# Zeros for 128 rows per expert once all tokens are counted, places read straight from TensorE's counts, and all gates computed at the end

## Time and profile before

| | us |
|---|---|
| runs | 1171.95, 1174.45, 1176.95 (median 1174.45) |
| the profiled execution, device time | 1172.36 |
| its span, first to last instruction | 1170.7 |
| TensorE busy | 1045.8 (89%) |
| VectorE busy | 577.0 (49%) |
| ScalarE busy | 484.0 (41%) |
| GpSimd busy | 306.9 (26%) |

### The profile page before, as it was taken

The page is one execution under the profiler, slowest core; times in us unless marked ns, Lnnn a source line. Parts: engine busy times, 40 slices in busy tenths (PEclk is TensorE's granted clock), DMA queues, the critical chain, the costliest instruction groups (busy, mean ns, idle before and its releaser), DMA issues.

```text
span 1170.7 us, 15177 instructions
## 1 busy us (share of the span) xinstructions
PE 1045.8 (89%) x4960; PEld 738.7 (63%) x4961; DVE 577.0 (49%) x1140; ACT 484.0 (41%) x1094; POOL 306.9 (26%) x309
## 2 busy tenths in 40 slices
PE   4999798897209999999999999499999999999998
PEld 3667575574204444444444444389999999999997
DVE  3775867757401111111111111697777777777764
ACT  5776666663100111111111111575555555555554
POOL 5665655743020000000000000432323232232222
PEclk9999999998658999999999999699999999999999
DMA  8554554505691444103491110200101000010000
GB/s 204 133 141 137 157 140 139 146 23 157 247 369 47 180 180 165 50 34 130 170 373 37 36 36 18 63 2 1 54 1 54 1 24 32 1 55 1 28 1 27
DMA packets 52758, 110.95 MB, mean 95 GB/s; under 512 B 7256, under 2 KB 16472, under 8 KB 52184
## 3 DMA queue, kind: packets, MB, share of 16 engines
q1 hardware_dynamic: 44104, 87.35, 23.5%
q0 software_dynamic: 4992, 16.26, 4.3%
q10 hardware_dynamic: 3600, 6.56, 1.4%
HBM read 82.36 MB, written 27.79 MB: 94 GB/s over the span
## 4 chain that ended last, share of the span: by engine, by line
PE 66%; DVE 2%; issue 1%; DMA 1%; POOL 1%; ACT 0%; POOLq 0%; DVEq 0%
PE scores L1294 15%; PE average L1302 15%; PE scores L1345 5%; PE scores L1347 5%; PE scores L1346 5%; PE average L1360 2%; PE mix L1361 2%; PE turned L1360 2%; PE scores L1309 2%; PE average L1361 2%; PE turned L1361 2%; PE mix L1360 2%; PE average L1359 2%; PE turned L1359 2%; PE mix L1359 2%
## 5 line engine op out<-in xcount | busy, mean ns | idle before, releaser
L1294 PE MATMUL scores<-w_sb,xt 128*128 x400 | 178.6, 600 | 2.3 <-issue 1.4
L1302 PE MATMUL average<-w_sb,hidt 128*128 x400 | 175.9, 593 | 1.0 <-DVE hidt L1009 1.0
L526 POOL TENSOR_TENSOR g_lo<-g,g_hi 128x384 fp32r<-128x384 f32 x96 | 98.2, 1023 | 290.4 <-ACT g_hi L728 290.4
L1345 PE MATMUL scores<-yt_hi,w_in_hi 128*128 128x384 f32 x384 | 132.4, 345 | 1.2 <-DVE yt_lo L1030 1.2
L1294 PEld LDWEIGHTS scores<-w_sb,xt 128*128 128x128 f32 x400 | 75.1, 193 | 88.2 <-issue 88.2
L1347 PE MATMUL scores<-yt_hi,w_in_lo 128*128 128x384 f32 x384 | 130.2, 339 | 0.0
L1346 PE MATMUL scores<-yt_lo,w_in_hi 128*128 128x384 f32 x384 | 130.0, 339 | 0.0
L1302 PEld LDWEIGHTS average<-w_sb,hidt 128*128 128x128 f32 x400 | 74.1, 190 | 84.9 <-issue 84.9
L1051 DVE COPY_PREDICATED ser<-big,th 128x384 f32<-128x384 int32 x96 | 118.8, 1238 | 3.3
L683 ACT ACTIVATE hid<-scores 128x512 f32<-128x512 f32 x50 | 29.9, 597 | 218.1 <-PE scores L1294 218.1
L1004 DVE COPY xt<-turned 128x512 f32<-128x512 f32 x26 | 18.0, 692 | 206.0 <-PE turned L1284 206.0
(11 more groups left out here) (231 smaller groups left out, 2077.6 us busy)
## 6 DMA issues: line engine op xcount, KB each, us to landing
w_sb<-in_w SPq DMA_DIRECT2D x14, 2048.0 KB, 13.8
q_sb<-in_qt SPq DMA_DIRECT2D x48, 288.0 KB, 4.1
x_sorted<-zeros SPq DMA_DIRECT2D x8, 1408.0 KB
k_sb<-in_kt SPq DMA_DIRECT2D x32, 288.0 KB, 4.3
xin<-x_sorted POOLq DMA_DIRECT2D x26, 256.0 KB, 2.9
y_sorted<-y_sb ACTq DMA_DIRECT2D x25, 256.0 KB, 2.0
v_sb<-in_v SPq DMA_DIRECT2D x16, 256.0 KB, 2.6
w_sb<-in_w SPq DMA_DIRECT2D x8, 512.0 KB, 3.8
```

The lines of the kernel that those rows point to most:

```text
L526: pool.tensor_tensor(g_lo[:, t % GRING, :], g32[:, t % 2, :], g_hi[:, t % GRING, :].bitcast(F32), ALU.subtract).then_inc(g_lo_ok, 1)
L1294: last = mm(s_ps[0][j][:, :], xt[:, c, :], w1_sb[:, r, c, j * 512:(j + 1) * 512], start=c == 0, stop=c == CD - 1)
L1302: last = mm(o_ps[0][:, :], hidt[:, c, :], w2_sb[:, r, c, :], start=c == 0, stop=c == CF - 1)
L1345: mm(ff_h(t), w_h, yt_hi[:, j % 2, c, :], start=c == 0, stop=False)
```

## The change

- `fill` writes 128 rows for each expert instead of 704, in one DMA with one row for each partition. It runs once all four batches are counted (`r_fill`, set after the last batch's rows), not after three.
- GpSimd scatters the last batch without waiting for the fills; the wait for `filled` stands behind these scatters, ahead of the tile loads.
- SyncE loads w1 of expert 1 once x is complete, then come the fills, then w2 of expert 1 and both of expert 2.
- All `turn_x` of a batch stand at the end of a step: tiles 0 and 1 at i = 4 of half 0, tile 2 at i = 3 and tiles 3 and 4 at i = 4 of half 1. ScalarE copies all five. The scores of i = 2 and 3 in half 1 and half 2 wait for these copies.
- Logits (tiles 0 and 1 in half 1, tiles 2 to 4 in half 2, at i = 2) and counts (half 3, i = 2) are no longer inside `turn`; they go to free columns of the `mix` bank. VectorE reads them there itself: `take_logits` at i = 2 of half 2, `place_rows` at i = 2 of half 3. `back(n - 1, 0)` waits for these reads.
- `pick` has four steps (and the maximum in `take_logits`) and stands at the end of i = 4 of half 2; the one-hot rows are bf16 from the start, the mask is in the compared numbers.
- `count` adds up everything in PSUM: the triangle product, a product with ones for each earlier tile of the batch, and one with a carried sum of all earlier batches (each expert's base is its first term), so that a row number is one product with the one-hot rows and one sum. `count_so_far` (two steps, end of i = 4 of half 3) makes the carried sum; `rows_of` stands at the end of i = 3. For the last batch one more column block gives the totals.
- `gate_of` and ScalarE's exponentials for it are gone from the loop; all 20 tiles' gates are computed in one pass after the table.
- The scatters of a batch stand between GpSimd's additions: tiles 0 and 1 in half 3, tiles 2 to 4 in the next half 0; of batch 2, tiles 2 to 4 ahead of the additions of iteration 16.

The core of the diff:

```diff
-                row = sp.value_load(fill_i[0:1, e:e + 1], min_val=0, max_val=E * REG + P - FILL)
-                sp.dma_start(xs[bass.ds(row, FILL), :].rearrange("(p t) d -> p t d", t=8),
-                             zeros[0:FILL // 8, None, :].to_broadcast([FILL // 8, 8, DM])).then_inc(filled, 16)
+                row = sp.value_load(fill_i[0:1, e:e + 1], min_val=0, max_val=E * REG)
+                sp.dma_start(xs[bass.ds(row, P), :], zeros[:, :]).then_inc(filled, 16)
...
-            sp.wait_ge(r_rows, B - 1)
+            expert_ready(0)
+            sp.wait_ge(x_ok, NP * QT)
+            load_w1(1, w_ok[1])
+            sp.wait_ge(r_fill, 1)
             for e in range(E):
                 fill(e)
-            expert_ready(0)
-            sp.wait_ge(x_ok, NP * QT)
-            for e in range(1, RING):
-                load_expert(e, w_ok[e])
+            load_w2(1, w_ok[1])
+            load_w1(2, w_ok[2])
+            load_w2(2, w_ok[2])
...
-                if n == NP - 1:
-                    for i in range(QT):
+                if n == NP:
+                    for i in range(2, QT):
                         scatter(B - 2, i)
+                b, pair = divmod(n - PAIRS, PAIRS)
                 if 1 <= n <= NP:
                     for i in range(QT - 1):
                         add(n - 1, i)
-                b, pair = divmod(n - PAIRS, PAIRS)
-                if 0 <= b < B - 2 and pair == PAIRS - 1:
-                    for i in range(3):
-                        scatter(b, i)
-                if 1 <= b < B - 1 and pair == 0:
-                    for i in range(3, QT):
-                        scatter(b - 1, i)
-            pool.wait_ge(filled, 16 * E)
+                        if 0 <= b < B - 1 and pair == PAIRS - 1 and i in (1, 2):
+                            scatter(b, i - 1)
+                        if 1 <= b < B - 1 and pair == 0 and i < QT - 2:
+                            scatter(b - 1, i + 2)
             for i in range(QT):
                 scatter(B - 1, i)
+            pool.wait_ge(filled, 16 * E)
             pool.wait_ge(zero_out, 16)
...
+                    if 0 <= b < B - 1 and half == 0 and i == QT - 1:
+                        move_x(b * QT, s_ps[(m + 1) % 2][1])
+                        move_x(b * QT + 1, s_ps[m % 2][1])
+                    if 0 <= b < B - 1 and half == 1 and i == QT - 2:
+                        move_x(b * QT + 2, s_ps[m % 2][1])
+                    if 0 <= b < B - 1 and half == 1 and i == QT - 1:
+                        move_x(b * QT + 3, s_ps[(m + 1) % 2][1])
+                        move_x(b * QT + 4, s_ps[m % 2][1])
...
+            def take_logits(b, bank, a):
+                dve.wait_ge(logit_ok, 2 * (b + 1) if b < B - 1 else 2 * b + QT)
+                dve.tensor_copy(L[:, b * QT:(b + 1) * QT, :], bank[:, a:a + 2 * E * QT].rearrange("p (i e) -> p i e", e=2 * E)).then_inc(l_ok, 1)
+                dve.wait_ge(l_ok, b + 1)
+                rs(dve.tensor_reduce(small[:, 0, :], L[:, b * QT:(b + 1) * QT, 0:E], AX.X, ALU.max))
...
+                d = r_d[:, b * QT:(b + 1) * QT, :]
+                dve.tensor_tensor(d, L[:, b * QT:(b + 1) * QT, 0:E], small_m, ALU.subtract).then_inc(r_diff, 1)
+                dve.wait_ge(r_diff, b + 1)
+                rs(dve.scalar_tensor_tensor(r_a[:, :, :], d, 0.0, desc[:, None, :].to_broadcast(full), ALU.is_equal, ALU.mult))
+                rs(dve.tensor_reduce(small[:, 1, :], r_a[:, :, :], AX.X, ALU.max))
+                dve.tensor_tensor(hots(b), desc_v[:, :, :], small_h, ALU.is_equal).then_inc(r_hot, 1)
+                dve.wait_ge(r_hot, b + 1)
...
+            def place_rows(b, bank, a):
+                dve.wait_ge(r_count, b + 1)
+                dve.tensor_tensor(r_a[:, :, :], bank[:, a:a + QT * E].rearrange("p (i e) -> p i e", e=E), hots(b), ALU.mult).then_inc(r_ranks, 1)
                 dve.wait_ge(r_ranks, b + 1)
...
+            def rows_of(b):
                 rs(dve.tensor_reduce(row_f[:, 0, b * QT:(b + 1) * QT], r_a[:, :, :], AX.X, ALU.add))
-                if b == B - 2:
-                    dve.tensor_copy(fill_i[:, :], inc[:, :, QT])
-                dve.tensor_copy(tot[:, :, 0], inc[:, :, QT])
                 dve.tensor_copy(row_u[:, b * QT:(b + 1) * QT], row_f[:, 0, b * QT:(b + 1) * QT]).then_inc(r_rows, 1)
...
+            def count_so_far(b):
+                rs(dve.tensor_reduce(sum_e8[:, :], hot[:, 0:(b + 1) * QT + 1, :].rearrange("p g e -> p e g"), AX.X, ALU.add))
+                dve.tensor_copy(carry[:, :], sum_e8[:, :]).then_inc(r_carry, 1)
...
+                    if 0 <= b < B - 1 and i == 2 and half == 2:
+                        take_logits(b, m_ps, LOGITS)
+                    if 0 <= b < B - 1 and i == 2 and half == 3:
+                        place_rows(b, m_ps, RANKS)
...
+                    if 0 <= b < B - 1 and i == 4 and half == 2:
+                        pick(b)
+                    if 0 <= b < B - 1 and i == 4 and half == 3:
+                        count_so_far(b)
+                    if 0 <= b < B - 1 and i == 3 and half == 3:
+                        rows_of(b)
+            take_logits(B - 1, t_ps[1], 0)
             pick(B - 1)
-            place_rows(B - 1)
+            place_rows(B - 1, t_ps[0], 0)
+            rows_of(B - 1)
+            dve.tensor_copy(base_n[:, :], t_ps[0][:, QT * E:(QT + 1) * E])
+            rs(dve.tensor_copy(fill_i[:, :], t_ps[0][:, QT * E:(QT + 1) * E]))
+            dve.sem_inc(r_fill, 1)
...
+            dve.wait_ge(r_exp, 2)
+            rs(dve.tensor_reduce(sum_e, r_e[:, :, :], AX.X, ALU.add))
+            rs(dve.tensor_scalar(sum_e, sum_e, 1e-9, None, ALU.add))
+            rs(dve.reciprocal(sum_e, sum_e))
+            rs(dve.tensor_scalar(r_b[:, :, :], r_b[:, :, :], 1.0, None, ALU.add))
+            rs(dve.reciprocal(r_b[:, :, :], r_b[:, :, :]))
+            rs(dve.tensor_tensor(r_b[:, :, :], r_b[:, :, :], hot[:, 1:TILES + 1, :], ALU.mult))
+            rs(dve.tensor_reduce(sum_b, r_b[:, :, :], AX.X, ALU.add))
+            rs(dve.tensor_tensor(gate[:, :], sum_e, sum_b, ALU.mult))
...
+            def count(b, bank, a, tiles):
+                pe.wait_ge(r_hot, b + 1)
+                if b:
+                    pe.wait_ge(r_carry, b)
+                mm(bank[:, a:a + QT * E], trib[:, :], hot[:, b * QT + 1:(b + 1) * QT + 1, :].rearrange("p g e -> p (g e)"), start=True, stop=False)
+                if tiles > QT:
+                    mm(bank[:, a + QT * E:a + tiles * E], onesb[:, :], hot[:, (b + 1) * QT, :], start=False, stop=False)
+                for j in range(QT - 1):
+                    mm(bank[:, a + (j + 1) * E:a + tiles * E], onesb[:, :],
+                       hot[:, b * QT + 1 + j, None, :].to_broadcast([P, tiles - 1 - j, E]), start=False, stop=False)
+                before = carry[:, None, :] if b else hot[:, 0:1, :]
+                mm(bank[:, a:a + tiles * E], onesb[:, :], before.to_broadcast([P, tiles, E]), start=False, stop=True).then_inc(r_count, 1)
...
+                    if routed and half in ROUTE and i in (1, 2):
+                        pe.wait_ge(xl_act, b * QT + (0 if half == 1 else 3) + i)
...
+                    if routed and half in ROUTE and i == 2:
+                        pe.wait_ge(first_moved, n)
+                        logits_of(b, half)
+                    if routed and half == 3 and i == 2:
+                        pe.wait_ge(first_moved, n)
+                        count(b, m_ps, RANKS, QT)
...
+                            if routed and half == 2:
+                                pe.wait_ge(l_ok, b + 1)
+                            if routed and half == 3:
+                                pe.wait_ge(r_ranks, b + 1)
...
+                    if routed and half == 0 and i == 4:
+                        turn_x(b * QT, s_ps[(m + 1) % 2][1])
+                        turn_x(b * QT + 1, s_ps[m % 2][1])
+                    if routed and half == 1 and i == 3:
+                        turn_x(b * QT + 2, s_ps[m % 2][1])
+                    if routed and half == 1 and i == 4:
+                        pe.wait_ge(xl_act, b * QT + 3)
+                        turn_x(b * QT + 3, s_ps[(m + 1) % 2][1])
+                        turn_x(b * QT + 4, s_ps[m % 2][1])
```

More of the change, by code:

```diff
@@ L119, in build @@
         started2 = sb("started2", [P, SLOTS + 1, E], F32)
-        small = sb("small", [P, 8, QT], F32)
+        small = sb("small", [P, 2, QT], F32)
+        sum_g = sb("sum_g", [P, 2, TILES], F32)
         small_e = sb("small_e", [P, 8, E], F32)
@@ L432, in q_rest @@
                 pool.wait_ge(k_split, n + 1)
[L433 to L435 removed]
+                b, pair = divmod(n - 2 * PAIRS - 1, PAIRS)
+                if b >= 0:
+                    pool.wait_ge(scattered, 16 * (b * QT + (2 if pair == 0 else QT)))
                 pool.tensor_tensor(q_st[D:P, p, :, 0:S], q2_sb[D:P, p, :, :], q_st[D:P, p, :, 0:S].bitcast(F32),
@@ L884, in place_rows, with hots @@
-            def place_rows(b):
```

(48 more changed lines are left out.)

191 lines of the change are left out of this document (42 added, 149 removed).

## The result

The changed kernel takes 1124.86 us (median of 4 runs, 1122.72 to 1125.72) against 1175.7 beside it; the ratio is 0.9568, with a 95% interval of 0.9539 to 0.9598. The profiled execution took 1122.72 us, 49.6 less than the one before. 1130 was forecast.

The account below looks back on a forecast made before the run. TensorE was taken as nearly full except near 300 to 350 us, waiting on late scatters and the first expert tile's load. 1172.4 - 30.1 - 14.0 = 1128.3, the median 2.1 above that execution: 1130 us, range 1118 to 1146.

Parts of the forecast that it names:

- The fills: Between attention and experts: smaller fills, scatters not waiting for them, first expert tile loaded at 321.2 instead of 351.35: minus 30.1 us.
- Attention: In the pairs with routing: TensorE's waits go, less returning VectorE steps and a longer count: minus 14.0 us, bounds 0 to 20.9.
- The wait term: In attention: waits of 20.9 us for one-hot rows, gate steps and turned x go, 5.4 us come back.
- the stall at the pair's end: Picking, summing and row steps on VectorE at pair ends cost 1.8 us for each of three batches, 5.4 us in all.
- a longer count: In attention, the count has five to six products instead of two: 1.5 us more over three batches.
- that stretch at half clock: In attention after the gate steps: if it goes with the stall, up to 1.7 us more for two; left in the range.
- A: Rival: only the wait between attention and experts shrinks, attention gains nothing or a third: 1144 or 1140 us; chance 0.21.
- B: Rival: fills overlap badly, each waiting out its landing, 3.4 us each, 27 us for eight: 1146 us; chance 0.08.
- C: Rival: no stall returns in attention, two half-clock stretches go, tile load lands 2 us sooner: 1122 us; chance 0.06.
- D: Rival: fills cost per transfer and wait for each other's landing, 8.75 us each, 70 us for eight: 1189 us; chance 0.03.
- The expected marks: Profile signs: first scatter 8 us and first expert product 27 us after last x tile, that tile at 281, fills within 11.
- One sign of being wrong: In attention: pairs half 1 to 3 still above 17 us would show the forecast wrong.

Follow-up runs that it names:

- e4: The changed kernel with four of its eight fills issued on ScalarE's queue instead of SyncE's: 1124.57 us against 1126.03 beside it.
- e7: The changed kernel with w2 of expert 1 and both weights of expert 2 issued only once the first expert tile has landed: 1121.88 us, ratio 0.9556.
- e6: The kernel before without gate steps in the attention pairs, all 20 tiles' gates in one pass behind the table, old fills: 1170.66 us, ratio 0.997.
- e1: The kernel before with only the new 128-row fills, w1 of expert 1 ahead and last scatters not waiting for them: 1146.97 us, ratio 0.9776.
- e5: The changed kernel with picking and summing steps moved from a pair's end to behind the next pair's last mixed tile: 1120.94 us, ratio 0.9545.
- e9: The changed kernel with steps behind the last mixed tile, four fills on ScalarE's queue and later weights behind the first tile's load: 1114.86 us, ratio 0.9514.

## Why the prediction was right

**The fills (30.1 forecast, 28.2 measured).** The mechanism was as forecast, but for which of two ends comes last. Row numbers: 7.4 us behind the last x tile, forecast 7.7. Fills: from 281.3 to 292.2 us, 10.9 us for eight, 1.36 each instead of the 1.0 that I took; the load of a row number took 0.27 to 0.58 us on SyncE's queue. The last landed 2.25 us later (2.4 forecast), at 294.08, 20.4 us behind the last x tile. By the forecast the fills were to land at 18.5 us and the scatters, at 19.6, to decide. The last scatter, at 287.37, would have released GpSimd at about 293.5 (an estimate with the median of the earlier trace rows; e4 gained only 0.6 us there). So the fills decided, 0.9 us later than the forecast end. The tile's load took 6.50 us, not 5.43; e7 shows that this is the weights' traffic, with 3.01 us without it. These two terms, +0.9 and +1.1, are the whole miss. With the fills alone the kernel gained 27.5. One term that came to nothing in the sum was not constant: the first tile's 16 products, 9.72 us before and kept so in the forecast, took 8.56 here and 9.69 and 9.63 in the two further profiles.

**Attention (14.0 forecast, 21.0 in the profile).** The wait term was right: 29.7 - 14.5 = 15.2 us of waits went, forecast 20.9 - 5.4 = 15.5, and the stall at the pair's end came back at 5.1 us, forecast 5.4 (picking 1.2 each, summing 0.5 each). The 1.5 us for a longer count was too much: its six products take 0.31 us of TensorE in the first batch (126.91 to 127.22 us), the two before took 0.21. The step that was mis-sized most is the one that I left in the range: "if that stretch at half clock goes with the stall, it is up to 1.7 us more for two of them; I leave it in the range". The clock was a term of its own. Over the whole of attention the mean granted clock read 0.96 before, and 1.00 in the changed kernel's first profile:

```profile
33.00:294.70 261.70, 229.75 (x1627) 164.12 (x1627) 187.26 (x536) 163.14 (x431) 147.14 (x137) 0.96 0.47 132
```

Against the window of the changed kernel above (240.60 us, TensorE busy 223.34) this gives the sum: TensorE was idle 31.95 us and is idle 17.26, 14.7 less, and it is busy 6.4 us less, although it has no less to compute. That second part is the clock.

Six short stretches at 1.2 GHz stand in the trace before, not two. Four begin within 1.5 us behind a stall of VectorE's making (the three of the gate steps, ended at 142.27, 214.41 and 285.93 us, and one for the one-hot rows, ended at 265.12); two begin near the end of the 24 narrow products of the logits (164.93 to 167.68 and from 237.01), with TensorE busy. That the gate stalls call the stretches up is not shown: e6 is without these stalls and has six as well. How many occur is partly chance. The changed kernel profiled again had two each time; in the third set they lie in the last two of these windows:

```profile
33.00:276.00 243.00, 225.87 (x1648) 162.51 (x1647) 174.86 (x493) 166.12 (x421) 147.47 (x137) 0.99 0.46 127
235.00:245.00 10.00, 10.00 (x75) 8.77 (x73) 4.04 (x10) 6.23 (x14) 4.55 (x3) 0.83 0.06 21
262.00:272.00 10.00, 7.32 (x36) 3.41 (x36) 5.22 (x23) 0.54 (x1) 6.76 (x9) 0.83 0.33 118
```

Its last x tile was complete at 275.99 us instead of 273.63, with the same waits: 1.2 us for each such stretch. The second set has 276.17 us, and e4 and e7, with the same attention and two stretches each, 276.98 and 276.83: up to 1.7 us each. So the first profile was a lucky one. Attention is worth about 18.6 us with two stretches, the usual case in these profiles, and 21.0 with none.

**The sum.** 1.9 us less in the hole, 7.0 more in attention: 5.1 more in all by the profiles. The median is as far off, 1124.86 against 1130; there the kernel before took 1175.7 us where the forecast started from 1174.45.

**The rivals.** A (only the hole closes): e1 is that kernel, 1147; out. B (fills that wait out their landing, 3.4 us each): 1.36 each; out. The page of the Trainium skill on DMA, "DMA: Bandwidth & Descriptors" (section "Anatomy of one DMA"), has about 2.0 us plus the bytes at 436 GB/s for a transfer issued from GpSimd, which makes an estimated 2.6 us for 256 KB. Here the fills are SyncE's: one landed in 2.25 to 2.3 us, a little sooner, and eight in a row took 1.36 us each, all but the issue overlapped, so the sum of 21 us for eight did not come. C (no stall comes back): the stall did come back; e5 takes it out, 5.1 us more. D (8.75 us a fill): out.

**The expected marks.** First scatter 7.7 us behind the last x tile (8 forecast). First work on the expert tile, its transpose, 28.7 us behind it (27 forecast, and 57 before, which is the transpose too; the first product by w1 came at 30.7). Last x tile at 273.6 (281). Two marks were missed: at most 1 us for a mixed tile at a pair's end, measured 1.2 behind picking, and the fills over within 11 us of the rows, where the last was issued 11.1 us behind them and landed at 13.0. One sign of being wrong was touched: of the eleven windows by pair, two that hold the turned x of a batch and its logits are 17.2 us long and one 17.1, with the limit at 17.

## What to carry to other kernels

Put small steps of a helper engine behind the last result that the bounding engine waits for in that round, not at the end of the round's program order: the same steps cost 5.1 us at one place and nothing one step later. Price the clock as a term of its own, from a window of the granted clock over the whole stage and from more than one profile, not from one dip; and do not count on a stretch at low clock to go with the stall ahead of it (e6). And when a large wait goes, look at once at the two next ends behind it: here fills and scatters landed within 1 us of one another, and the load behind both was slowed by transfers that nobody needed yet.

## What the runs showed of the hardware

- A short stretch at half clock in attention costs 1.2 to 1.7 us (last x tile at 273.63 us with none, at 275.99 to 276.98 in four profiles with two), and the same program had none in one execution and two in others (0.83 over the two windows above).
- Such stretches come in two places in the trace before: four within 1.5 us behind a stall of 2.1 to 2.8 us, two near the end of 24 narrow products with TensorE busy.
- A transfer of 256 KB that lands in 2.9 to 3.0 us alone (e7, e9) takes 6.1 to 6.9 us beside 6.3 MB of queued weight loads, though these were issued 1.7 to 3.4 us earlier on another queue.
